# Four buffers for the raw weights of the first tile, and the last stores of x one by one between weight loads

## The reference

```python
a = softmax(phi)                                  # (8, 8, 576, 32)
k_m, v_m = einsum(a, k), einsum(a, v)             # 32 memory slots per head
x = softmax(q @ k_m.T / 8) @ v_m                  # 4608 tokens of 512
h = x @ w_in;  x2 = (h * sigmoid(1.702 * h)) @ w_out      # d_ff 2048
e = argmax(x2 @ w_gate)                           # 8 experts, one per token
out = gate(x2) * eom(x2) * relu(x2 @ w1[e]) @ w2[e]       # d_ff 1024
```

## Time and profile before

| | |
|---|---|
| three plain runs | 1346.61 us median (1345.87 to 1348.1) |
| profiled execution | 1348.39 us, its span 1346.8 us |
| mean granted TensorE clock | 0.994 of full |
| PE busy | 1309.3 us, 97% of the span |
| POOL busy | 554.6 us, 41% |
| DVE, ACT busy | 634.2 us (47%), 388.6 us (29%) |
| SP's DMA queue (q1) | 204.30 MB, 43.6% of 16 engines' span |

### The profile page before, as it was taken

One profiled execution on the slowest core, in us unless ns is written; L12 is line 12 of the kernel. 1 busy time (PEld: TensorE's weight loads), 2 busy tenths in 40 slices (PEclk: granted clock), 3 DMA queues, 4 the chain that ended last, 5 costly groups with the idle time before them and its releaser, 6 DMA issues.

```text
span 1346.8 us, 23538 instructions
## 1 busy us (share of the span) xinstructions
PE 1309.3 (97%) x6866; PEld 1054.9 (78%) x6867; DVE 634.2 (47%) x1291; ACT 388.6 (29%) x725; POOL 554.6 (41%) x648
## 2 busy tenths in 40 slices
PE   5997999999999999999999999999999999999997
PEld 3455888888888888888888888887788888888886
DVE  4893243443533434334334343447555555555553
ACT  3672222222222322222222222223322222222221
POOL 2455764454434442443444334512443242433332
PEclk9998999999999999999999999999999999999999
DMA  9996357555565464654654546557874778549872
GB/s 362 401 423 233 103 179 204 200 195 173 200 185 188 168 195 156 186 188 164 178 191 168 189 164 177 185 175 234 255 206 99 224 236 257 161 135 266 238 241 63
DMA packets 152924, 274.26 MB, mean 204 GB/s; under 512 B 16947, under 2 KB 54084, under 8 KB 150308
## 3 DMA queue, kind: packets, MB, share of 16 engines
q1 hardware_dynamic: 96100, 204.30, 43.6%
q10 hardware_dynamic: 43584, 37.37, 11.4%
q0 software_dynamic: 13184, 31.88, 7.4%
HBM read 144.98 MB, written 100.45 MB: 182 GB/s over the span
## 4 chain that ended last, share of the span: by engine, by line
PE 90%; DMA 4%; DVE 2%; issue 1%; POOL 1%; SPq 1%; ACT 0%; ACTq 0%; POOLq 0%
PE ps L699 29%; PE ps L733 28%; PE ps L774 15%; PE ps L803 15%; DMA phT<-in_phi 3%; PE ps L743 1%; DMA raw<-in_moe_w_out 1%; DMA raw<-in_moe_w_in 1%; DVE sc L1150 0%; DVE scs L1152 0%; DVE scs L1161 0%; PE ps L618 0%; PE ps L671 0%; POOL W L1541 0%; DMA cq<-ch 0%
## 5 line engine op out<-in xcount | busy, mean ns | idle before, releaser
L699 PE MATMUL ps<-xs,W 128*128 (+1 forms) x1728 | 420.1, 392 | 5.1 <-POOL W L1541 5.1
L733 PE MATMUL ps<-W,gs 128*128 128x512 f32 x1728 | 415.4, 389 | 1.2 <-POOL W L1531 1.1
L699 PEld LDWEIGHTS ps<-xs,W 128*128 128x128 f32 x1728 | 324.5, 189 | 75.2 <-issue 8.2
L733 PEld LDWEIGHTS ps<-W,gs 128*128 128x128 f32 x1728 | 324.5, 188 | 69.4 <-issue 1.5
L1225 DVE TENSOR_TENSOR gate<-ps,gate 128x512 f32<-128x512 f32 x144 | 99.5, 691 | 373.5 <-ACT gate L969 373.1
L969 ACT ACTIVATE gate<-ps 128x512 f32<-128x512 f32 x144 | 86.1, 598 | 474.9 <-PE ps L699 459.6
L803 PE MATMUL ps<-W,chT 128*128 (+1 forms) x936 | 218.2, 389 | 1.0 <-DVE chT L1362 0.8
L774 PE MATMUL ps<-W,cx 128*128 (+1 forms) x936 | 218.5, 389 | 0.5 <-issue 0.5
L1595 POOL CAST whi<-raw 128x512 fp32r<-128x512 f32 x128 | 83.6, 653 | 317.2 <-DMA raw<-in_moe_w 317.2
L803 PEld LDWEIGHTS ps<-W,chT 128*128 128x128 f32 x936 | 175.6, 188 | 38.1 <-issue 1.8
L774 PEld LDWEIGHTS ps<-W,cx 128*128 128x128 f32 x936 | 175.6, 188 | 37.4 <-issue 1.1
(11 more groups left out here) (163 smaller groups left out, 781.3 us busy)
## 6 DMA issues: line engine op xcount, KB each, us to landing
W<-expert_scratch SPq DMA_DIRECT2D x24, 2048.0 KB, 10.3
raw<-in_moe_w SPq DMA_DIRECT2D x128, 256.0 KB
expert_scratch<-whi SPq DMA_DIRECT2D x128, 256.0 KB, 2.6
expert_scratch<-raw SPq DMA_DIRECT2D x128, 256.0 KB, 2.8
cq<-ch ACTq DMA_DIRECT2D x156, 128.0 KB
kvm<-in_kv SPq DMA_DIRECT2D x16, 1152.0 KB, 10.6
crec<-record_scratch POOLq DMA_DIRECT2D x160, 64.0 KB
qT<-in_q SPq DMA_DIRECT2D x16, 576.0 KB, 8.6
```

What stands on the lines that cost most here:

```text
L699: mm = pe.matmul(ps[:, f % 2, :], W[:, col:col + P], xs[:, bass.ds(x0 + (x_lo * K1 + c) * T, T)], start=(c == 0 and w_lo + x_lo == 0), sto ...
L733: mm = pe.matmul(ps[:, 2 + s, :], gs[:, f % 2, g_lo, s * P:(s + 1) * P], w_out_sb[:, f, w_lo, :], start=(f == 0 and g_lo + w_lo == 0), sto ...
```

## The change

Two more raw buffers, `raw2`, are laid where `kvm2` lies in stage A and `whi` in stage B; for that, `xo` moves onto the buffers `qT0` and `kvm0`, and a few other tiles of stage A move. Loads 4, 5, 6, 7 and on use the four buffers in turn. Loads 6 and 7 are issued ahead of the big stores, when the K and V sums of group 14 are done (`s_kv` at 15), which is when the last group that used `kvm2` has read it. From load 8 on, SP waits for `s_wlo` at n - 3. The four small stores are issued singly, each behind one of the loads 8 to 11, and `load_x` behind them. POOL's waits follow the four semaphores. Nothing is computed in another way.

```diff
+            xo = sbt(a, "xo", [P, 2, 2, S])
+            raw2 = sbt(a, "raw2", [P, 2, CH])
...
-        s_wraw = [sem(f"w_raw_loaded{u}") for u in range(2)]
+        s_wraw = [sem(f"w_raw_loaded{u}") for u in range(4)]
...
+        w_raw = [raw[:, 0, :], raw[:, 1, :], raw2[:, 0, :], raw2[:, 1, :]]
+
+        def w_slot(n):
+
+            return n % 2 if n < K1 else n % 4
+
+        def w_loads(n):
+
+            return n // 2 + 1 if n < K1 else (n - K1) // 4 + 1 + (2 if w_slot(n) < 2 else 0)
...
-            def store_kept(b, n, stored):
+            def store_kept(b, n, stored, us=range(2)):
 
                 sp.wait_ge(s_xo, 4 * (b + n))
-                for u in range(2):
+                for u in us:
...
             def load_w(n, src):
 
-                wait(sp, s_wlo, n - 1)
-                sp.dma_start(raw[:, n % 2, :], src).then_inc(s_wraw[n % 2], 16)
+                if n in (K1 + 2, K1 + 3):
+                    sp.wait_ge(s_kv, NG - 1)
+                else:
+                    wait(sp, s_wlo, n - 1 if n < K1 + 2 else n - 3)
+                sp.dma_start(w_raw[w_slot(n)], src).then_inc(s_wraw[w_slot(n)], 16)
...
-            load_w(K1, w_out_v[0])
-            load_w(K1 + 1, w_in_part(0, 1))
+            for c in range(2):
+                load_w(K1 + 2 * c, w_out_v[c])
+                load_w(K1 + 2 * c + 1, w_in_part(c, 1))
             store_kept(0, FIRST, s_xfirst)
-            for b in range(FIRST, KEPT):
-                store_kept(b, 1, s_xkept)
...
                     for k in range(1, 4):
                         for c in range(K1):
                             f = 4 * (k - 1) + c
-                            if f:
+                            if f >= 2:
                                 load_w(K1 + 2 * f, w_out_v[f])
+                                if f < 4:
+                                    store_kept(FIRST + f - 2, 1, s_xkept, (0,))
                                 load_w(K1 + 2 * f + 1, w_in_part(c, k))
+                                if f < 4:
+                                    store_kept(FIRST + f - 2, 1, s_xkept, (1,))
...
-                pool.wait_ge(s_wraw[i], 8 * (n - i) + 16)
-                pool.tensor_copy(hi, raw[:, i, :]).then_inc(s_whi, 1)
+                pool.wait_ge(s_wraw[w_slot(n)], 16 * w_loads(n))
+                pool.tensor_copy(hi, w_raw[w_slot(n)]).then_inc(s_whi, 1)
```

More of the change, by code:

```diff
@@ L145, in build, with load_buffers @@
             sbt(a, "before_xs", [P, 2560 - 4 * 2 * D - 3 * S - 6 * (SB + 2) - 2 * D])
-            def load_buffers(u):
+            def load_buffers(a, u):
                 return (sbt(a, f"qT{u}", [P, QA // 2, HG, M]), sbt(a, f"kvm{u}", [P, QA * D * 2]), sbt(a, f"phT{u}", [P, S]))
-            q1, kv1, ph1 = load_buffers(1)
+            q1, kv1, ph1 = load_buffers(a, 1)
             sbt(a, "to_512_first", [P, 64])
-            q0, kv0, ph0 = load_buffers(0)
-            sbt(a, "to_512_second", [P, 64])
+            with ExitStack() as a2:
+                q0, kv0, ph0 = load_buffers(a2, 0)
+            xo = sbt(a, "xo", [P, 2, 2, S])
+            sbt(a, "before_aT", [P, K1 * T * 2 - 4 * S])
             aT = sbt(a, "aT", [P, S])
@@ L159, in build @@
             kvs = sbt(a, "kvs", [P, 2 * D])
-            kv2 = sbt(a, "kvm2", [P, QA * D * 2])
+            with ExitStack() as a2:
+                kv2 = sbt(a2, "kvm2", [P, QA * D * 2])
+            sbt(a, "before_raw2", [P, 6 * T - 2 * S - P - 2 * D])
+            raw2 = sbt(a, "raw2", [P, 2, CH])
             pT.append(sbt(a, "pT1", [P, S]))
             sbt(a, "to_512_third", [P, 64])
[L163 to L167, removed]
+            q2 = sbt(a, "qT2", [P, QA // 2, HG, M])
+            ph2 = sbt(a, "phT2", [P, S])
             qT, kvm, phT = [q0, q1, q2], [kv0, kv1, kv2], [ph0, ph1, ph2]
@@ L1523, in _, with split_w @@
         def _(pool):
-            def split_w(n, i, f):
+            def split_w(n, f):
                 hi, lo = w_out_sb[:, f, 0, :], w_out_sb[:, f, 1, :]
-                pool.wait_ge(s_wraw[i], 8 * (n - i) + 16)
-                pool.tensor_copy(hi, raw[:, i, :]).then_inc(s_whi, 1)
+                pool.wait_ge(s_wraw[w_slot(n)], 16 * w_loads(n))
+                pool.tensor_copy(hi, w_raw[w_slot(n)]).then_inc(s_whi, 1)
                 pool.wait_ge(s_whi, n + 1)
-                pool.tensor_tensor(lo, raw[:, i, :], hi.bitcast(F32), ALU.subtract).then_inc(s_wlo, 1)
+                pool.tensor_tensor(lo, w_raw[w_slot(n)], hi.bitcast(F32), ALU.subtract).then_inc(s_wlo, 1)
             def split_w_in(n, c, k):
-                i = n % 2
-                by_f = raw[:, i, :].rearrange("p (f n) -> p f n", f=4)
+                by_f = w_raw[w_slot(n)].rearrange("p (f n) -> p f n", f=4)
                 hi, lo = w_in_sb[:, 4 * k:4 * k + 4, 0, c, :], w_in_sb[:, 4 * k:4 * k + 4, 1, c, :]
-                hold(pool, s_wraw[i], 8 * (n - i) + 16)
+                pool.wait_ge(s_wraw[w_slot(n)], 16 * w_loads(n))
                 pool.tensor_copy(hi, by_f).then_inc(s_whi, 1)
-                hold(pool, s_whi, n + 1)
+                pool.wait_ge(s_whi, n + 1)
                 pool.tensor_tensor(lo, by_f, hi.bitcast(F32), ALU.subtract).then_inc(s_wlo, 1)
@@ L1618, in pool_tile @@
                                 kept_stored(pool)
-                            split_w(K1 + 2 * f, 0, f)
+                            split_w(K1 + 2 * f, f)
                             split_w_in(K1 + 2 * f + 1, c, k)
                     for f in range(12, C1):
-                        split_w(16 + f, f % 2, f)
+                        split_w(16 + f, f)
                     pool.wait_ge(b_cst, 16)
```

## The result

| | before | changed | difference |
|---|---|---|---|
| plain runs, median (range) | 1346.54 us (1345.82 to 1348.10) | 1338.89 us (1337.88 to 1341.02) | -7.65 |
| profiled execution | 1348.39 us | 1339.29 us | -9.10 |
| its span, mean clock | 1346.8 us, 0.994 | 1337.6 us, 0.998 | -9.2 |

The ratio is 0.994, 95% interval 0.9929 to 0.9951. Two later comparisons with more runs of before gave 0.9934 (0.9921 to 0.9947) and 0.9929 (0.9916 to 0.9943), with 9.31 and 9.33 us between the medians.

A forecast was written before the change was run, and what follows sets the result against it. PE, 97% busy, was bound by first-tile waits for POOL's splits, held by late loads, plus slow clock: 1.30 + 0.10 + 5.22 + 2.70 = 9.32 us, off the median 1346.61 gives 1337.3 us; own range 1336.0 to 1338.5, widened 1335.5 to 1341.

The forecast's parts named there:

- The hole at mm2(0,1): First tile: PE's wait for split 6, 1.30 us, would go because loads 6 and 7 precede the big stores.
- The hole at mm1(0,4): First tile: 5.22 us lost ahead of mm1(0,4), waiting for split 11, would go.
- slow clock: First tile, after the wait at mm1(0,4): matmuls at the lower clock cost 2.70 us, which would go too.
- The throttled time times a half: Other pricing of the slow clock in the first tile: 6.8 us at half level, 3.4 us lost, 10.0 in all.
- Three us to spare at split 11: POOL's split 11 would end at 116.7 to 119.5; PE wants it at 122.55 for mm1(0,4).
- The late big stores: SP queue: big stores issued at about 90.7 instead of 84.44, costing nothing, at most some 1 us of empty queue.
- at worst all of it goes ahead of load 11: DMA queue: ACT's whole xo store (1.18 MB) served first would make load 11 land at 117.5, not 114.6.
- the first rival: Transfers share the engines, leaving 2.0 us of hole at mm1(0,4), perhaps 2.7 more; gain 4.6 to 7.3 us; chance 0.13.
- The gate: ScalarE's wait for all stores, after step 2: last lands at some 119, may open until 122.5, no cost.
- The rival "slower": Last small store holds ScalarE at its gate past 122.5; 0.2% slower if it lands at 131.8; chance 0.04.
- VectorE beside POOL: VectorE's subtraction at L1227, 0.94 us longer beside POOL's splits, would end at 113.76, before mm2(0,1) at 114.39: no cost.
- The pace at mm1(0,8): 20 splits due at 144.3: done at 138 to 142, or 143.1 even at POOL's present 2.72 us a split.

The follow-up runs named there:

- the other execution of before: The kernel before with no edit, run again as a control: median 1347.45 us, and 1235.1 us from the start of mm2(0,0) in its profile.

## Why the prediction was right, point by point

**The hole at mm2(0,1), 1.30 us.** Right: splits 6 and 7 run on without a gap, and mm2(0,1) follows mm2(0,0) at once. Buffers alone, with load 6 still behind the stores, bring the wait back at 1.23 us.

**The hole at mm1(0,4), 5.22 us, and 2.70 us of slow clock.** Right: mm1(0,5) is 127.89 - 111.54 = 16.35 us behind mm2(0,0), where the prediction has 16.32. From mm2(0,0) the two profiles differ by 9.0 us, against 9.3 forecast. The plain medians differed by 7.65 in the first comparison and by 9.3 in two later ones, so the first, at 1338.89, lies 1.6 us over the 1337.3 forecast and 0.4 outside the forecast's own range of 1336.0 to 1338.5. The throttled time times a half would have given 10.0; priced from the matmuls' starts the slow clock is 2.70, and 1.95 in the other execution of before. In both it is half of the time that PE worked at the low level, within 0.1 us: 5.6 us (129.17 to 134.7) and 3.9 us (128.05 to 132.0).

**Three us to spare at split 11: mis-sized.** "Load 11 to 114.6 ... at worst ... 117.5" came out as 109.81 + 10.3 = 120.1, and the split at 122.13, with 0.3 to 2.4 us to spare in three executions. Two terms failed.

The late big stores were to cost "nothing", at most "some 1 us" of empty queue: the window at 90 us carried 285 GB/s and not 434, which is 5 x 0.149 = 0.75 MB, or 1.8 us at 0.41 MB/us, and the window at 85 us another 0.23 MB, so some 2.4 us in all (some 1.8 in the two other profiles of the changed kernel, whose two windows add up to 694 and 698 against 844 in the other one of before). The reason given was that load 5 lands only at 92.1, so that the engines have work until then. It landed at 91.5 (84.15 + 7.3), but the engines had fallen to 250 GB/s from 89 to 90 us and to 98 from 90 to 91: the landing of the last load isn't the time until which they are full.

The other term: "at worst all of it goes ahead of load 11" was not the worst: from 95 us on the queue ran at the rate I took (385 to 429 GB/s by window), so from 95 to 120 it carried 10.25 MB, where I had counted 9.90 from the big stores to load 11, so at least 0.35 MB that I had placed behind load 11 came out ahead of it. The store of xo, issued at 109.47, took 10.5 us, so it landed at 120.0, ahead of load 11. SP was late as well, though less: the issues from 103 on took 0.8 to 1.5 us each, and the x load went out at 112.44, not near 110.

The slack that I left covered both terms with 0.3 us left in this execution, which was partly luck; had it been thinner, the first rival would have come true.

**The gate.** Right in kind, mis-sized too: the last store landed at 121.5, not 119, and the gate opened 0.9 us ahead of the 122.5 that I worked out. The rival "slower" is a real mechanism: with the stores behind load 15 it gave back nearly all of the gain, at the place and with the slow clock as described.

**VectorE beside POOL.** Right: 1.56 us for 0.69, no cost, since it ended at 113.56 against 114.26 for mm2(0,1).

**The pace at mm1(0,8).** In the changed kernel split 19 ended at 141.7, 2.5 us before mm1(0,8) at 144.21. My remark that even the present pace of 2.72 us a split would do was too bold: it started from a split 12 that ends at 124.1, and split 12 ended at 126.8, from where 2.72 us a split would have made mm1(0,8) 1.7 us late. With two buffers, and split 12 ending at 129.3, mm1(0,8) waited 1.97 us.

## What to carry to other kernels

In a stretch where the DMA queue is full, a load's price is what stands ahead of it, so put the loads that an engine will wait for ahead of stores that nobody waits for soon. Whether the stores then stand singly between the loads or in a block behind the last load that matters made no difference from mm2(0,0); that the medians of the two kernels with the block lie 1.2 to 1.6 us higher is not explained. Of the 9.3 us the buffers alone gave 4.6, the small stores behind loads alone 3.7, and early loads with the buffers 5.4; early loads without the buffers were not tried. Each of them shortens or removes a hole and leaves, or opens, another. When stores move back, look for every gate that counts their landing; moving such a gate to a later step took back the 6 us that late stores had cost at the early one.

## What the runs showed of the hardware

A hole in PE's work doesn't always bring the slow clock, and its length alone doesn't decide it. After 1.95 us idle (buffers only) and 2.83 us (single stores only) the granted clock stayed at 1.00. After 2.70 us (early loads and buffers) it fell all the same, at 124.4, when PE had been at work again for 0.9 us; in the second wait, of 1.65 us, it was back at 1.00. After 5.06, 5.16 and 5.91 us each time the next steps ran slow, at a cost of 2.70, 1.95 and 2.8 us, and there the clock fell within the hole, 3.8, 2.3 and 4.8 us after PE had stopped.

An issue on SP takes 0.33 to 0.43 us as a rule, 0.35 too at 102.85 in the changed kernel, where the engines carry 429 GB/s. But the issues from 103.25 to 115.52 take 0.8 to 1.64 us each. The two big stores took 2.33 us together in two profiles of the changed kernel and 0.94 in the third. A busy queue alone isn't the reason then; what is, no run here separates.
